# Reading the first expert layer and the last matrix with four neighbouring rows in one partition

## The reference

```python
# 1. attention with a local window and 8 global keys: B, H, S, Dh = 4, 8, 768, 64
x = attention(q, k, v).transpose(0, 2, 1, 3).reshape(3072, 512)
# 2. soft mixture of experts: E = 8 experts, 4 slots each, phi [512, 32], w1 [8, 512, 1024], w2 [8, 1024, 512]
logits = x @ phi
d = softmax(logits, axis=0); c = softmax(logits, axis=1)
slot_input = (d.T @ x).reshape(8, 4, 512)
for e in range(8):
    slot_out[e] = np.maximum(slot_input[e] @ w1[e], 0) @ w2[e]
y = c @ slot_out.reshape(32, 512)
# 3. squared-relu layer: w_in [512, 2048], w_out [2048, 512]
out = np.maximum(y @ w_in, 0) ** 2 @ w_out
```

## Time and profile before

| | |
|---|---|
| median of 3 runs | 506.81 us (506.44 to 506.99) |
| the profiled execution | 506.44 us |
| its span | 504.6 us |
| busy share of the span | PE 95%, DVE 72%, ACT 69%, POOL 19% |
| mean granted TensorE clock | 0.996 of full speed |
| HBM read | 70.39 MB |

### The profile page before, as it was taken

The page is one execution under the profiler, slowest core; times in us unless marked ns, Lnnn a source line. Parts: engine busy times, 40 slices in busy tenths (PEclk is TensorE's granted clock), DMA queues, the critical chain, the costliest instruction groups (busy, mean ns, idle before and its releaser), DMA issues.

```text
span 504.6 us, 12853 instructions
## 1 busy us (share of the span) xinstructions
PE 480.8 (95%) x4608; PEld 398.9 (79%) x4608; DVE 363.3 (72%) x1026; ACT 346.3 (69%) x761; POOL 94.8 (19%) x223
## 2 busy tenths in 40 slices
PE   2999999999999998799899999999999999999996
PEld 1667677777667643337789999999999999999996
DVE  6687877787787661318989978777687777768782
ACT  2788897897898610016999887776777776777740
POOL 1555454545445403300000000000000000000000
PEclk9999999999999999989999999999999999999999
DMA  7699889884565799993001011010110101001011
GB/s 284 255 348 361 353 307 336 320 311 166 193 202 189 279 350 410 420 400 129 1 0 44 2 43 42 0 42 0 42 42 0 42 0 42 21 21 42 0 43 42
DMA packets 17979, 77.24 MB, mean 153 GB/s; under 512 B 2320, under 2 KB 2320, under 8 KB 14352
## 3 DMA queue, kind: packets, MB, share of 16 engines
q1 hardware_dynamic: 14720, 60.95, 32.8%
q10 hardware_dynamic: 3216, 15.73, 8.1%
HBM read 70.39 MB, written 6.29 MB: 152 GB/s over the span
## 4 chain that ended last, share of the span: by engine, by line
PE 80%; ACT 9%; DVE 5%; issue 3%; POOL 1%; DMA 1%; DVEq 0%; ACTq 0%; POOLq 0%
PE bank L1629 14%; PE bank L1628 14%; PE bank L1630 14%; ACT probs L1027 5%; PE bank L1288 5%; PE bank L1600 4%; PE bank L1276 4%; PE bank L1303 4%; PE bank L1557 3%; PE bank L1530 3%; PE bank L1308 2%; PE bank L1349 2%; PE bank L1328 2%; POOL probs L463 1%; DVE probs L553 1%
## 5 line engine op out<-in xcount | busy, mean ns | idle before, releaser
L1027 ACT ACTIVATE probs<-probs,nmax 128x232 f32<-128x232 f32 (+1 forms) x192 | 88.6, 463 | 31.0 <-DVE nmax L553 30.1
L463 POOL TENSOR_SCALAR probs<-probs,rden 128x232 f32<-128x232 f32 (+1 forms) x192 | 82.9, 452 | 88.6 <-DVE rden L562 88.6
L1628 PE MATMUL bank<-t_hi,s_hi 128*128 128x256 f32 x352 | 98.7, 280 | 0.0
L1629 PE MATMUL bank<-t_lo,s_hi 128*128 128x256 f32 x352 | 98.6, 280 | 0.0
L1630 PE MATMUL bank<-t_hi,s_lo 128*128 128x256 f32 x352 | 98.5, 280 | 0.0
L1150 ACT ACTIVATE g_s<-bank 128x1024 f32<-128x1024 f32 x48 | 48.9, 1022 | 30.2 <-PE bank L1600 30.2
L1179 ACT ACTIVATE s_hi<-s 128x512 fp32r<-128x512 f32 x88 | 55.0, 627 | 18.4 <-DVE s L954 14.6
L1628 PEld LDWEIGHTS bank<-t_hi,s_hi 128*128 128x128 f32 x352 | 66.5, 189 | 0.0
L1629 PEld LDWEIGHTS bank<-t_lo,s_hi 128*128 128x128 f32 x352 | 66.4, 189 | 0.0
L1630 PEld LDWEIGHTS bank<-t_hi,s_lo 128*128 128x128 f32 x352 | 66.4, 189 | 0.0
L877 DVE TENSOR_TENSOR s_lo<-s,s_hi 128x512 fp32r<-128x512 f32 x88 | 56.9, 687 | 6.8 <-DVE s L954 3.5
(11 more groups left out here) (194 smaller groups left out, 1025.8 us busy)
## 6 DMA issues: line engine op xcount, KB each, us to landing
qkv_s<-qkv_dram SPq DMA_DIRECT2D x15, 1028.0 KB, 7.3
qkv_s<-qkv_dram SPq DMA_DIRECT2D x16, 704.0 KB, 5.4
w_s<-w_dram ACTq DMA_DIRECT2D x5, 2048.0 KB, 12.0
w_s<-w_dram SPq DMA_DIRECT2D x13, 512.0 KB, 8.6
out_dram<-o_stage SPq DMA_DIRECT2D x24, 256.0 KB, 2.0
wo_raw<-w_out_dram SPq DMA_DIRECT2D x4, 1024.0 KB, 14.5
w_a<-w_dram SPq DMA_DIRECT2D x3, 1024.0 KB, 11.7
w_a<-w_dram SPq DMA_DIRECT2D x5, 512.0 KB, 6.4
```

What stands on the lines that cost most here:

```text
L463: last = pool.tensor_scalar(probs[:, v % 2, m, a, 0:w], probs[:, v % 2, m, a, 0:w], rden[:, v % 2, m, a:a + 1], 1.0, ALU.mult, ALU.mult)
L1027: act.activation(probs[:, v % 2, m, a, 0:w], probs[:, v % 2, m, a, 0:w], ACT.Exp, bias=nmax[:, v % 2, m, a:a + 1], scale=-1.0, accum_out=d ...
L1628: pe.matmul(OUT[n], hi, W_HI[n](at_f), start=(c == 0 and f == 0 and n in (0, 2, 4, 5)), stop=False, skip_group_check=True)
L1629: pe.matmul(OUT[n], hi, W_LO[n](at_f), start=False, stop=False, skip_group_check=True)
```

## The change

All of `w1` and of `w_out` is read with four neighbouring rows in one partition: partition p gets rows 4p to 4p + 3. A whole expert's first layer is then one run of 16 KB in each partition, and a quarter of `w_out` one of 8 KB. The features in a partition must agree on the other side: the product that makes `si_t` takes every fourth column of `slot_acc`, and the copies of `mix` read PSUM with a step of four elements instead of two. The loads into the places of experts 1 to 3 become three parts (chunk 0, chunks 1 and 2, chunk 3) of three loads each instead of four parts.

```diff
+        W1_PARTS = ((0, 1), (1, 3), (3, 4))
...
-        w1_part = [sem(f"w1_part{c}") for c in range(DC)]
+        w1_part = [sem(f"w1_part{n}") for n in range(len(W1_PARTS))]
...
-        w1_v = w1.rearrange("e (c p) f -> e p c f", p=P)
+        w1_v = w1.rearrange("e (p c) f -> e p c f", p=P)
...
         def mix_blocks(n):
-            return mix[:, n * 512:(n + 1) * 512].rearrange("p (i r q) -> p i r q", i=2, r=2)
+            return mix[:, n * 512:(n + 1) * 512].rearrange("p (r q) -> p r q", r=4)
...
-            for c, m in enumerate(("l1_0_0", "l1_0_1", "l1_0_2", "l1_0")):
-                sp.wait_ge(mid_pe, pe_at[m])
+            for n, (c0, c1) in enumerate(W1_PARTS):
+                sp.wait_ge(mid_pe, pe_at[("l1_0_0", "l1_0_2", "l1_0")[n]])
                 for j in range(1, 4):
-                    sp.dma_start(w1_s[j][:, c, :], w1_v[4 + j, :, c, :]).then_inc(w1_part[c], 16)
+                    sp.dma_start(w1_s[j][:, c0:c1, :], w1_v[4 + j, :, c0:c1, :]).then_inc(w1_part[n], 16)
...
-                sp.dma_start(wo_raw[:, blocks, :].rearrange("p (i r) n -> p i r n", r=2),
-                             w_out.rearrange("(i p r) n -> p i r n", p=P, r=2)[:, 2 * n:2 * n + 2, :, :]).then_inc(wo_in[n], 16)
+                sp.dma_start(wo_raw[:, blocks, :],
+                             w_out.rearrange("(i p r) n -> p i r n", p=P, r=4)[:, n, :, :]).then_inc(wo_in[n], 16)
...
-                dve.tensor_copy(mix_blocks(n), bank[4 + n][:, :].rearrange("p (i q r) -> p i r q", i=2, r=2)).then_inc(mix_dve, 1)
+                dve.tensor_copy(mix_blocks(n), bank[4 + n][:, :].rearrange("p (q r) -> p r q", r=4)).then_inc(mix_dve, 1)
...
             for c in range(DC):
-                if c == DC // 2:
+                if c == 0:
                     dve("slot_acc_1")
-                last = pe.matmul(bank[2][:, c * SLOTS:(c + 1) * SLOTS], slot_acc[SG, c * P:(c + 1) * P], fold_n[SG, :])
+                last = pe.matmul(bank[2][:, c * SLOTS:(c + 1) * SLOTS], slot_acc[SG, bass.ds(c, P, step=DC)], fold_n[SG, :])
...
-                                if (g, j) == (1, 1):
-                                    pe.wait_ge(w1_part[c], 48)
+                                if (g, j) == (1, 1) and c in [c0 for c0, _ in W1_PARTS]:
+                                    pe.wait_ge(w1_part[[c0 for c0, _ in W1_PARTS].index(c)], 48)
```

More of the change, by code:

```diff
@@ L1141, in _ @@
                 act.wait_ge(mid_pe, pe_at[f"m{n}"])
-                act.activation(mix_blocks(n), bank[4 + n][:, :].rearrange("p (i q r) -> p i r q", i=2, r=2), ACT.Copy).then_inc(mix_act, 1)
+                act.activation(mix_blocks(n), bank[4 + n][:, :].rearrange("p (q r) -> p r q", r=4), ACT.Copy).then_inc(mix_act, 1)
             def relu(G, c, u, spent=None):
```

## The result

| | before | changed |
|---|---|---|
| median | 506.84 us (505.47 to 508.41, 10 runs) | 509.39 us (507.68 to 511.37, 10 runs) |
| the profiled execution, its span | 506.44, 504.6 us | 509.56, 507.8 us |
| mean granted clock in it | 0.996 | 0.993 |

The ratio is 1.0047 [1.003, 1.0064]. The change makes the kernel 0.5% slower, outside the predicted range and on the side to which I gave 0.13. All ratios here leave slow executions out (one of 2138 us of changed_again, one of 531 us of the kernel before beside it), and they are not the plain quotients of the two medians.

The account below looks back on a forecast made before the run. PE, busy 95%, was held by a DMA-throughput hole before group 1's second layer. Only a 0.2 us earlier landing counted, other terms nothing or absorbed: 506.44 - 0.2 = 506.2 profiled, median 506.6, range 504.7 to 507.7.

Parts of the forecast that it names:

- What bounds the kernel: PE's 3.25 us hole before group 1's second layer, set by DMA throughput; half speed behind it lost 1.3 us.
- The step of four in `slot_acc`: Strided weight loads of the product for `si_t`: taken as 0, between 0 and 0.42 us, which would fall into the hole.
- PE is 0.44 late up to the hole; there it is absorbed, because the DMA wait ends last: PE's lateness from waiting for `slot_acc_1` was to vanish in the hole before group 1's second layer, costing nothing.
- SP's later issues: `w1` requests for experts 5 to 7 go out 0.44 later; `w2_part[0]` up to 0.5 us later, taken as nothing.
- The wait: All weight loads for `si_t` now wait for DVE's `slot_acc_1`, so they start 0.44 us later.
- Bytes and landings: 8 KB runs for 3 of 6 MB of `w1` land `w2_part[0]` 0.2 us earlier; bounds 0 to 1.0 more.
- `mix`, `w_out`, attention: Copies with step four, `w_out` landing 0.3 us earlier, and attention loads: each taken as nothing; `mix` at most 1.0 near the path.
- Rival 4: Slower: queue runs dry around chunk 0, `w2_part[0]` up to 0.5 us later, 507.3 us; chance 0.09.
- Rival 1: The clock stays up through a hole 0.75 us shorter, returning 1.3 us: 505.3 us; chance 0.26.
- Rival 2: The `w1` queue loses its hesitation, `w2_part[0]` lands up to 1.2 us earlier, clock stays: 504.3 us; chance 0.10.
- Rival 3: Slower: 16 KB runs hold back five attention loads, stalling PE's scores by 2 us: 508.8 us; chance 0.07.

Follow-up runs that it names:

- changed_again: The changed kernel measured once more, without any further edit: 508.69 us, ratio 1.0038 to the kernel before.
- the ladder: Kernel before plus 16 unread products behind `si_t`, four each with weight steps 1, 2, 3 and 4; only weight-load durations were compared, no median given.
- the four parts: Changed kernel with the step of four in DVE's reads and `w1` asked for in four parts, twelve loads in 4 KB runs: 507.5 us, ratio 1.0026.
- w_out_alone: Kernel before with only the edits of `w_out` (8 KB runs) and `mix` (copies with step four): 506.68 us, ratio 1.0014.
- step_on_dve: Changed kernel, but DVE reads PSUM with step four and writes `slot_acc` in chunk order, so weights are contiguous; wait kept: 507.76 us, ratio 1.0026.
- wait_alone: Kernel before with all products for `si_t` waiting for the second half of `slot_acc`, weights still contiguous: 507.55 us, ratio 1.0014.
- late_by_7_early: Kernel before with seven idle products (1.4 us) on PE ahead of group 0's first layer: 509.05 us, ratio 1.0048.

## Why the prediction was wrong

**What bounds the kernel**: right. The hole is a wait for bytes, and the half speed behind it was read rightly; moving one megabyte behind part 0 took 2.5 us from the landing.

**"The step of four in `slot_acc`"**: the first failed step. I put it at 0, with 0.42 as its bound, from the spacing of L1539's loads; it measured 0.97 in the span of the loads. The loads of the earlier trace rows are those of transposes, with another step, and neither their spacing nor their duration gave the price here. The duration, 193 against 140, was a sign that a step costs, and I set it aside for the spacing. The term was also bounded by a row with another step, as if the price at eight capped the price at four; the ladder gives 138 ns at four, where L1539 had suggested 53 at eight.

**"PE is 0.44 late up to the hole; there it is absorbed, because the DMA wait ends last"**: the second failed step, and the one that gives the sign. The landing isn't fixed in time. SP asks for `w1` when PE has done chunk 0 of group 0, so the whole queue starts with PE, and B is constant. Lateness ahead of that chunk passes to the landing one to one; behind it, it vanishes. Both halves are shown by the two kernels with seven idle products. I had the mark in the text under *SP's later issues* and worked out there that the queue had "at least nothing to spare", then still took nothing. One part of the mechanism stays open: the first `w1` load took 4.4 us behind `w2_c` and 3.6 in the empty queue of the changed kernel, so by that load alone 0.8 us of lateness should have been free, yet B is 29.35 and 29.37.

**The wait**: 0.50 against 0.44 forecast, right as a size. By itself it costs 0.5 us in A (4.03 for 3.53); the time, 1.0014 [0.9995, 1.0032], can't tell this from nothing.

**Bytes and landings**: 0.2 was forecast, about 0.4 measured in the landing of part 0 and nothing in that of part 3, and the reason given isn't shown, as the four parts tell.

**`mix`, `w_out`, attention**: right, nothing that shows (w_out_alone 1.0014 [0.9996, 1.0032]).

**Rivals.** Rival 4 has the right place, the queue that runs dry around chunk 0, and a far too small price: 0.5 where 2.7 came, since it counted only the wait. Rival 1 needs a shorter hole; step_on_dve (3.01) and changed_again (2.40) show holes without a fall, but w_out_alone kept its clock through one of 3.39 and wait_alone lost it behind one of 3.36, so the length alone doesn't decide. Rival 2's 1.2 earlier landing never came. Rival 3 is refuted: no new wait on an attention load.

**Not foreseen at all**: the fall of the clock in the first layer, which made up 1.07 of the 3.2 in the profiled pair, through the first chunk.

What stays open: what decides in which execution the clock falls, by what part 0 lands 0.4 us earlier in the new order of `w1`, and what else step_on_dve and late_by_7_early lose, about 1 us each. Of the 2.55 us between the medians, the wait (0.50), the weight loads (0.97) and the last product (0.16), less the 0.4 of the landing, make 1.2, and the additional falls 0.6; the other 0.7 isn't assigned.

## What to carry to other kernels

A DMA wait that ends last doesn't absorb lateness if the request for that DMA waits for the late engine: follow the landing back to the request, and the request to the work that it waits for, before calling anything hidden. A gather of every fourth element should stand where the trace shows it free: here in the copy of an engine that writes or reads the tile anyway (DVE 0.48 us, ACT 0.60 us for either order), and not in an operand of the matrix products. And where a queue is full, the order of its bytes is the lever: one megabyte sent behind what is wanted first gave 0.23%, where the longer runs gave nothing that shows; but a wait that is cut in one place can come back behind it, as here four chunks on.

## What the runs showed of the hardware

A weight load of 96 x 128 fp32, two to a product, takes 192, 196, 262 and 330 ns at steps 1, 2, 3 and 4; a moving operand of 256 fp32 columns at step four takes 627 instead of 385 ns. The granted clock fell from 2.4 to 1.2 GHz while PE was busy, 1.4 to 2.8 us after weight loads of 262 or 330 ns had begun, in each of four traces, and in none whose loads there took 192 ns. Elsewhere it fell in PE's holes of 1.97 to 3.36 us or up to 1.0 us behind them, when PE was at work again, and held through holes of 2.40, 2.43, 2.71, 3.01 and 3.39. A chain of 10 MB in one queue, with all later requests in time, took the same from the first request to its last landing wherever it started: 29.20 to 29.49 us in the old order, for requests from 185.75 to 193.05.
